# Layer norm's roots taken by way of DRAM, second-layer weight sums made early and kept in DRAM, operand forms moved to VectorE

## The reference

```
attn = softmax(masked q k^T / 8) v                     # 8 heads, local and strided masks
h = gelu(attn @ w_in);  u, v = halves of h
v_n = (v - mean) / sqrt(var + 1e-6) * g_ln
x = attn + (u * (w_sg @ v_n + b_sg)) @ w_out
mu, var = mean and variance of x over its 512 features
xn = (x - mu) / sqrt(var + 1e-6) * g_ln2               # the layer norm of the title
out = x + relu(xn @ w_ch1) @ w_ch2                     # 512 -> 2048 -> 512
```

## Time and profile before

| | |
|---|---|
| median of 3 runs | 750.08 us (749.67 to 751.82) |
| the profiled execution's own time | 746.97 us |
| its span, first to last instruction | 745.2 us |
| PE busy | 677.8 us (91%) |
| DVE, ACT, POOL busy | 551.9, 364.3, 272.4 us |
| mean granted TensorE clock | 0.966 |
| moved by DMA | 82.37 MB, 31.6% of 16 engines' span |

### The profile page before, as it was taken

How to read it: one execution, slowest core, us unless ns; L and a number is a source line. 1 busy time by engine, 2 the same in 40 slices (tenths; PEclk the granted TensorE clock), 3 DMA queues, 4 the chain that set the end, 5 groups by cost and what they waited for, 6 DMA issues and landing times.

```text
span 745.2 us, 14093 instructions
## 1 busy us (share of the span) xinstructions
PE 677.8 (91%) x5158; PEld 635.7 (85%) x5160; DVE 551.9 (74%) x1288; ACT 364.3 (49%) x896; POOL 272.4 (37%) x262
## 2 busy tenths in 40 slices
PE   8899999899989999994689599989966999999998
PEld 4579888898789889994579489989966999999997
DVE  6877967996799776864346557646679979799794
ACT  6756747485647643342253244334555444344441
POOL 1386332323142344755242233024993211212112
PEclk9999999999999999997799999999987999999999
DMA  8560016000700050051124221557540452724501
GB/s 299 196 216 1 1 56 226 1 1 2 279 1 2 2 178 1 29 184 60 49 72 132 92 80 64 188 195 256 177 136 31 159 191 65 286 67 179 190 29 48
DMA packets 41396, 82.37 MB, mean 111 GB/s; under 512 B 3440, under 2 KB 28912, under 8 KB 38640
## 3 DMA queue, kind: packets, MB, share of 16 engines
q1 hardware_dynamic: 41328, 81.48, 31.6%
HBM read 53.15 MB, written 28.31 MB: 109 GB/s over the span
## 4 chain that ended last, share of the span: by engine, by line
PE 57%; POOL 13%; issue 12%; DVE 10%; DMA 4%; ACT 3%; POOLq 0%; DVEq 0%; SPq 0%; ACTq 0%
PE pair L1693 9%; PE pair L1695 9%; PE pair L1694 9%; PE pair L1485 7%; PE pair L1487 7%; PE pair L1486 7%; DVE stage L1361 3%; PE pair L1509 3%; PE pair L1524 3%; PE pair L1542 2%; DMA hid_scratch<-stage 2%; POOL w_lo L481 2%; POOL acc L453 1%; DVE probs L1144 1%; DMA x_scratch<-res 1%
## 5 line engine op out<-in xcount | busy, mean ns | idle before, releaser
L1693 PE MATMUL pair<-xf_hi,w_hi 128*128 128x288 f32 x896 | 271.3, 303 | 26.9 <-POOL w_lo L481 6.8
L1694 PE MATMUL pair<-xf_lo,w_hi 128*128 128x288 f32 x896 | 268.5, 300 | 0.0
L1695 PE MATMUL pair<-xf_hi,w_lo 128*128 128x288 f32 x896 | 267.6, 299 | 0.0
L1693 PEld LDWEIGHTS pair<-xf_hi,w_hi 128*128 128x128 f32 x896 | 172.1, 192 | 31.1 <-issue 13.1
L1695 PEld LDWEIGHTS pair<-xf_hi,w_lo 128*128 128x128 f32 x896 | 172.8, 193 | 0.0
L1694 PEld LDWEIGHTS pair<-xf_lo,w_hi 128*128 128x128 f32 x896 | 172.4, 192 | 0.0
L1361 DVE TENSOR_TENSOR stage<-pair,stage 128x576 f32<-128x576 f32 x136 | 100.5, 751 | 65.0 <-PE pair L1695 32.7
L963 ACT ACTIVATE xf_hi<-res 128x576 fp32r<-128x576 f32 x140 | 94.1, 682 | 104.6 <-PE pair L1695 67.2
L522 DVE TENSOR_TENSOR xf_lo<-res,xf_hi 128x576 fp32r<-128x576 f32 x134 | 112.1, 854 | 26.3 <-ACT xf_hi L963 26.2
L1048 ACT ACTIVATE stage<-stage 128x576 f32<-128x576 f32 x64 | 43.5, 683 | 90.1 <-DVE stage L1361 90.0
L853 POOL TENSOR_TENSOR xr<-xr,stage 128x576 f32<-128x576 f32 x16 | 32.3, 2017 | 139.4 <-DVE stage L1361 139.4
(11 more groups left out here) (127 smaller groups left out, 1360.1 us busy)
## 6 DMA issues: line engine op xcount, KB each, us to landing
hid_scratch<-stage SPq DMA_DIRECT2D x64, 288.0 KB, 2.3
res<-hid_scratch SPq DMA_DIRECT2D x16, 1152.0 KB, 6.7
w_raw<-w_ff_dram SPq DMA_DIRECT2D x16, 512.0 KB, 3.8
v_sb<-vW_dram SPq DMA_DIRECT2D x16, 384.0 KB, 6.8
x_scratch<-res SPq DMA_DIRECT2D x4, 1152.0 KB, 5.1
xr<-x_scratch SPq DMA_DIRECT2D x16, 288.0 KB, 2.9
out_dram<-xr SPq DMA_DIRECT2D x16, 288.0 KB, 2.3
k_sb<-kT_dram SPq DMA_DIRECT2D x15, 304.0 KB, 6.7
```

The lines of the kernel that those rows point to most:

```text
L1693: pe.matmul(dst, wh, xh, start=(start and x == 0), stop=False)
L1694: pe.matmul(dst, wh, xl, start=False, stop=False)
L1695: last = pe.matmul(dst, wl, xh, start=False, stop=(stop and x == n - 1))
```

## The change

Four edits go together.

1. The variance leaves the chip's wide layout. ACT copies one row of the variance (1x288 for each half, `copy_variance`) instead of taking the root in all 128 partitions. POOL stores it to DRAM, loads it back as 96x6, adds epsilon and raises it to the power -0.5 in two small operations, stores the result and loads it spread over 128 partitions: four transfers for each norm, sixteen in all, issued by POOL. DVE's reciprocal is gone. The norms' last step is later: item 0's `normalise_x` is at the start of period 2, item 1's at the start of the last period, and those of items 2 and 3 both in lockstep 1 of the tile before they are used.
2. First-layer weights are loaded in parts: the blocks of P1 and P2 straight to their place (`f_raw`), that of P4 straight to its place, and the whole unit to `w_raw` for POOL's sums. All of it is issued ahead of the first hidden store.
3. The sums of second-layer weights are made by POOL in locksteps 4 to 11 in `w_raw` itself and stored to DRAM. In tile 3 each unit's P1 and P2 blocks are loaded as soon as P2 of the last lockstep that reads its place is done, and the rest, sums among it, after that lockstep.
4. All forms of x for the hidden layer and their splits are on DVE; POOL keeps four for the output layer.

Two statistics are one product later or earlier in PE's list. The diff, cut to its core:

```diff
-W_PLAIN = (P1, P2, P4)
-NPLAIN = len(W_PLAIN)
+W_FIRST = (P1, P2)
+NFIRST = len(W_FIRST)
+NREST = FORMS - NFIRST
+NSUMS = NREST - 1
...
-    place = {(1, P4): 0, (2, P1): 1, (2, P4): 2, (3, P7): 3}.get((q, i))
+    place = {(1, P4): 0, (2, P2): 1, (3, P1): 2, (3, P7): 3}.get((q, i))
...
-            if g >= UNITS:
-                engine.wait_ge(product_ready, ((B - 1) * LOCKSTEPS + u // 2 + 1) * FORMS)
-            elif u <= 1:
...
+            def load_raw(g):
                 if g >= 2:
-                    sp.wait_ge(plain_lo, g - 1)
-                    sp.wait_ge(w_sum, 4 * (g - 1))
+                    sp.wait_ge(w_sum, NSUMS * (g - 1))
                 sp.dma_start(w_raw[:, g % 2, :], w_ff[g]).then_inc(wff_in[g % 2], 16)
+
+            def load_first(g):
+                u = g % UNITS
+                if g < UNITS:
+                    wait_unit(sp, g)
+                else:
+                    sp.wait_ge(product_ready, ((B - 1) * LOCKSTEPS + u // 2) * FORMS + P2 + 1)
+                sp.dma_start(f_raw[u][:], w_ff[g, :, 0:NFIRST * BLOCK]).then_inc(f_in[u], 16)
+
+            def load_rest(g):
+                u = g % UNITS
+                if g >= UNITS:
+                    sp.wait_ge(product_ready, ((B - 1) * LOCKSTEPS + u // 2 + 1) * FORMS)
+                sp.dma_start(s_raw[u][:, 0:BLOCK], w_ff[g, :, NFIRST * BLOCK:(NFIRST + 1) * BLOCK]).then_inc(r_in[u], 16)
+                if g >= UNITS:
+                    sp.wait_ge(w2_stored, 16 * (u + 1))
+                    sp.dma_start(s_raw[u][:, BLOCK:NREST * BLOCK], sums_dram[u]).then_inc(r_in[u], 16)
+
+            def load_raw2(u):
+                if u == 0:
+                    sp.wait_ge(w_sum, NSUMS * UNITS)
+                else:
+                    sp.wait_ge(w2_sum, NSUMS * u)
+                sp.dma_start(w_raw[:, 0, :], w_ff[UNITS + u]).then_inc(w2_in, 16)
+
+            def store_sums(u):
+                sp.wait_ge(w2_sum, NSUMS * (u + 1))
+                sp.dma_start(sums_dram[u], w_raw[:, 1, :]).then_inc(w2_stored, 16)
...
-            for g in range(2, EARLY + 1):
-                load_unit(g)
+            for g in range(2, EARLY):
+                load_raw(g)
+                load_first(g)
+                load_rest(g)
+            for g in range(EARLY, EARLY + 2):
+                load_raw(g)
+                load_first(g)
+                load_rest(g)
             save_x(B - 1)
+            for g in range(EARLY + 2, UNITS):
+                load_raw(g)
+                load_first(g)
+                load_rest(g)
             for n in range(B):
                 for q in range(LOCKSTEPS):
                     m = n * LOCKSTEPS + q
-                    if n == 0 and q == 0:
-                        load_unit(EARLY + 1)
...
+                    if n == 0 and q == 3:
+                        load_raw2(0)
+                    if LOCKSTEPS < m <= LOCKSTEPS + UNITS:
+                        store_sums(m - LOCKSTEPS - 1)
+                        if m < LOCKSTEPS + UNITS:
+                            load_raw2(m - LOCKSTEPS)
+                    if n == B - 1 and q >= 1:
+                        load_rest(UNITS + 2 * q - 2)
+                        load_rest(UNITS + 2 * q - 1)
+                    if n == B - 1:
+                        load_first(UNITS + 2 * q)
+                        load_first(UNITS + 2 * q + 1)
...
+            def sum_second(u):
+                pool.wait_ge(w2_in, 16 * (u + 1))
+                if u == 0:
+                    pool.wait_ge(w_sum, NSUMS * UNITS)
+                else:
+                    pool.wait_ge(w2_stored, 16 * u)
+                add_blocks(pool, w_raw[:, 0, :], w_raw[:, 1, :], w2_sum, NSUMS * u)
+
+            def store_variance(n):
+                pool.wait_ge(var_copied, 2 * (n + 1))
+                pool.dma_start(var_dram[n:n + 1, :], norm_at(n)[0][0:1, :, :].rearrange("p h t -> p (h t)")).then_inc(var_stored, 16)
+
+            def load_variance(n):
+                pool.wait_ge(var_stored, 16 * (n + 1))
+                wait_past(pool, var_step, n)
+                pool.dma_start(var_c[:], var_dram[n].rearrange("(p x) -> p x", p=RP)).then_inc(var_in, 16)
+
+            def invert_roots(n):
+                pool.wait_ge(var_in, 16 * (n + 1))
+                wait_past(pool, pow_done, n)
+                pool.tensor_scalar(var_eps_c[:], var_c[:], EPS, None, ALU.add).then_inc(var_step, 1)
+                pool.wait_ge(var_step, n + 1)
+                wait_past(pool, rstd_stored, 16 * n)
+                pool.tensor_tensor(rstd_c[:], var_eps_c[:], half_c[:], ALU.pow).then_inc(pow_done, 1)
+                pool.wait_ge(pow_done, n + 1)
+                pool.dma_start(rstd_dram[n].rearrange("(p x) -> p x", p=RP), rstd_c[:]).then_inc(rstd_stored, 16)
+
+            def spread_rstd(n):
+                pool.wait_ge(rstd_stored, 16 * (n + 1))
+                if n == 1:
+                    pool.wait_ge(group_ready, (B - 1) * len(GROUPS))
+                to = gt[:, 0, :] if n == 1 else norm_at(n)[0][:].rearrange("p h t -> p (h t)")
+                pool.dma_start(to, rstd_dram[n:n + 1, :].broadcast_to([P, S])).then_inc(rstd_in, 16)
...
             def last_period(b):
-                pool.wait_ge(pv_ready, B * TWINS)
-                form_t3(pool, 0)
+                spread_rstd(1)
+                for g in range(2):
+                    sum_weights(g)
...
-                    if following < B and q == 3:
-                        form_t2(pool, following)
-                        split_form(pool, fill_of(following, P7))
-                        form_t1(pool, following)
-                        form_t4(pool, following)
-                        split_form(pool, fill_of(following, P3))
-                    if following == B and q >= 1:
-                        for g in (UNITS + 2 * q - 2, UNITS + 2 * q - 1):
-                            sum_weights(pool, g)
-                            split_plain(pool, g)
...
+                    if early and q == 0:
+                        sum_chunks(pool, r)
+                    if norm and q == 0:
+                        invert_roots(n + 1)
+                    if early and q == 1:
+                        split_sum(pool, r)
+                        sum_chunks(pool, r + 1)
+                    if early and q == 2:
+                        split_sum(pool, r + 1)
+                        sum_chunks(pool, r + 2)
+                        split_sum(pool, r + 2)
+                    if early and q == 3:
+                        sum_chunks(pool, r + 3)
+                        split_sum(pool, r + 3)
+                    if 0 <= u < UNITS:
+                        sum_second(u)
+                    if norm and q == 0:
+                        spread_rstd(n + 1)
+                    if early and q == 3:
+                        store_variance(n + 2)
...
+            def copy_variance(n, h):
+                r = 4 * n + 2 + h
+                act.wait_ge(stat_ready, r + 1)
+                if n == 1:
+                    act.wait_ge(xn_done, 2)
+                elif n == B - 1:
+                    act.wait_ge(xn_done, 2 * n)
+                act.activation(norm_at(n)[0][0:1, h, :], statistic_at(r)[0:1, :], ACT.Copy).then_inc(var_copied, 1)
...
-            def invert_root(n, h):
-                rstd = norm_at(n)[0]
-                dve.wait_ge(sd_done, 2 * n + h + 1)
-                dve.reciprocal(rstd[:, h, :], rstd[:, h, :]).then_inc(rs_done, 1)
-
             def normalise_x(n, h):
-                rstd = norm_at(n)[0]
-                dve.wait_ge(rs_done, 2 * n + h + 1)
+                dve.wait_ge(rstd_in, 16 * (n + 1))
+                dve.wait_ge(sq_done, (2 * n + h + 1) * KC)
+                wait_past(dve, xn_done, 2 * n + h)
...
+                if q == 3:
+                    split_form(dve, fill + 3)
+                if border:
+                    form_t1(dve, following)
                 c12(m)
+                if border:
+                    form_t4(dve, following)
+                    split_form(dve, fill + 4)
+                if last and q == 3:
+                    split_rest(dve, UNITS + 3)
+                c21(m)
...
+                if s in (0, 2, 4, 6):
+                    split_rest(dve, UNITS + 4 + s // 2)
```

438 lines of the change are left out of this document (223 added, 215 removed).

## The result

| | before | after |
|---|---|---|
| time, median of four runs each, us | 749.88 (749.55 to 751.82) | 729.78 (725.27 to 733.39) |
| ratio, 95% interval | | 0.9724, 0.9666 to 0.9782 |
| profiled execution, own time / span | 746.97 / 745.2 | 728.94 / 727.1 |
| DMA moved, MB | 82.37 | 98.26 |

A forecast was written before the change was run, and what follows sets the result against it. PE was taken as the engine to be fed before 568 us, losing 62.2 us to waits and slow clock. Terms -12.6 - 11.3 + 7 - 12.6 - 2 = -31.5 from 746.97 gave 715.5, plus 3.1 offset: 718.5 us, range 702 to 737.

The forecast's parts named there:

- Tile 0: Locksteps 1 to 3: earlier loads of units 6 and 7 cut the loss from 26.8 to 14.2 us, saving 12.6.
- where the clock holds it is 16.6: Upper case for the first tile's saving, without the 4 us of slow pace added for two gaps near 3.9.
- Tile 1: Second tile: shorter statistic waits and full clock cut the loss from 15.8 to 4.5 us, saving 11.3 (bounds 5 and 14).
- Tiles 2 and 3: Borders and transfers: loss grows from 4.0 to 11 us, 7 worse (bounds 2 and 14), with lockstep 11's gap becoming 5.5.
- The hops: Root's four POOL-issued transfers per norm, 2.5 us each, 10 in all, hidden before normalise_x with 5 us to spare.
- POOL's transfers are late: Rival, chance 0.15: at 5 us a hop, normalise_x stands 5 us in locksteps 5 and 9; 728.5 us in all.
- Output layer: Start of the output layer: both waits for second-layer weights go, loss 15.6 becomes 3, saving 12.6 us (bounds 8 and 14).
- Attention: Attention periods: less DVE work before first scores, less about 2.7 us of new waits; 2 us saved (bounds -4 and +6).
- a gap of up to 2.6 us costs itself: PE clock rule: such gaps add no slow pace, while gaps from 3.9 us up cost 3 to 6 us more.
- The first tile's stall only changes its name: Rival, chance 0.14: P1's copy behind its store is late by itself, so less is saved in the first two tiles; 733.5 us.
- slower: the stage store: Rival, chance 0.07: stage-1 stores land late in locksteps 4 to 15, PE idles 33.6 us and the gain is gone.
- The clock holds: Rival, chance 0.14: no gap reaches 3.9 us, so 4 and 3 us of slow pace don't come; 709 us.

The follow-up runs named there:

- e7: Changed kernel with the loads of first-layer units 6 and 7 late again, behind hidden stores of lockstep 0: 736.77 us, ratio 0.9825 to the kernel before.
- e10: Changed kernel with the statistics of the late items back in their old places (behind P1 and P4, not P2 and P1): 735.75 us, ratio 0.9805.
- e1: Changed kernel with the second half of normalise_x in locksteps 5 and 9 moved behind the last drain: 728.77 us, ratio 0.9697.
- e2: Changed kernel with GpSimd's sums of second-layer units 1 and 5 cut to 16 of 256 columns of a block: 727.32 us, ratio 0.9699.
- e0: The changed kernel timed again without edit, beside the kernel before: 732.52 us (727.91 to 738.09, six runs), ratio 0.9768.
- e6: Changed kernel with the early sums' transfers (raw second-layer loads, stores of sums) cut to 16 of 1024 columns: 725.85 us, ratio 0.9683.
- e9: Changed kernel with the four forms and the splits of P7 and P3 back on GpSimd at the three tile borders: 742.87 us, ratio 0.9887.
- e11: Changed kernel with five combined fixes, then hidden and x loads spread further and ScalarE's roundings of remainders moved later: 719.88 us, ratio 0.9594.
- e5: Changed kernel with the remainders of second-layer units 12 to 15 split in two pieces, the second four steps later: 734.24 us, ratio 0.9787.
- e3: Changed kernel with the remainders of second-layer units 14 and 15 split by GpSimd instead of VectorE: 731.7 us, median of five.
- e4: Changed kernel with three attention moves: first variance statistic one u group later, two normalise_x pieces later: 724.86 us, ratio 0.9669.

## Why the prediction was right, and where it was not

The time lies in the range, 11 us above the forecast's value and 3 above its own case (711 to 727), and terms were off on both sides. Tile 0 gained 4.3 us more than forecast, and tile 1 6.7, tiles 2 and 3 2.6, the output layer 5.9 and the attention 2.5 less. Only tile 0 offsets the others; it was the width of the range, 702 to 737, and not the terms, that made the hit.

*What bounds the kernel*: right. What moved lies ahead of 568 us, in PE's waits and the clock behind them; the rest took 138.2 us in both.

*Tile 0, 12.6 forecast, 16.9 measured.* The mechanism holds step by step. Unit 7 was to land at 328 to 331 (340.4 before) and ScalarE's rounding to come behind sums that end at 337 (345.81 before), and so they did:

```profile
329.56 0.75 POOL L482 TENSOR_TENSOR s_raw<-w_raw 128x256 f32<-128x256 f32 x1 [0.17 <-DMA w_raw<-w_ff_dram]
```

```profile
336.46 0.45 ACT L1028 ACTIVATE acc_hi<-acc 128x288 fp32r<-128x288 f32 x1 [2.13 <-POOL acc L464]
```

VectorE stands until 337.5 as forecast. The idle time is 6.5 us (1.88, 0.45, 0.94, 3.25) and not 10.2. The clock fell twice, behind 1.88 and behind 3.25, for 3.4 us each, so the slow pace of about 3.5 us came as forecast (4), and that the gain equals the bound "where the clock holds it is 16.6" is a coincidence: the clock did not hold. VectorE's stand behind the weight split, 3.4 us in the sum, cost 1.9. Wrong was that nobody but the roots waited for ACT's table loads: PE waited 1.96 us in lockstep 3 for a root behind one, and this wait went unpriced. e7 and e10 show the loads and the second mean's place as causes, with some 6.5 and 1.3 to 2.5 us; what the adds' order and the missing reciprocals add to that was not tried.

*Tile 1, 11.3 forecast, 4.6 measured: the step that failed.* The waits for statistics did shrink (3.91 to 0.94 and 0.26); where `normalise_x` holds PE up less, in e1 and e2, the second mean waits 2.44 and 2.43, which is the forecast's 2.3 to 2.7. But I left 4.5 us of loss for the tile and it has 11.2 (57.3 less 46.1), 8.0 of them idle. Two causes were not in the sum. Both halves of `normalise_x` stand in one lockstep with seven drains, and take 3.77 and 2.58 us beside GpSimd, where I counted two of 1.8 and no price for PE: gaps of 1.69 and 2.60 (e1, e2). And at the border VectorE's split is shut out by GpSimd's adds, 1.53. I had seen the contention on GpSimd's side (0.72 becoming 1.73) and not asked what it does to VectorE. The other 3.2 us are pace: the clock fell for 3.4 us behind the gap of 2.60, where I had put tile 1 at full clock.

*Tiles 2 and 3, +7 forecast, +9.6 measured (+12.8 in e0).* Lockstep 11 was right: 5.31 us of idle for 5.5, and the clock fell; e6 shows that the new megabyte makes 3.0 of it. What I had not counted are locksteps 9 and 10, 3.7 us over before, 3.2 of it gaps: `normalise_x` again, and roots that came late. The two borders there, 1 us each in the sum, cost nothing (locksteps 8 and 12 take 11.2).

*The hops: sized well and hidden in one tile out of two.* The four hops in tile 0's chain took 10.1 us (2.3, 1.9, 1.9 and 3.9) for the forecast's 10, and ended 6.7 us before VectorE took them up. In tile 1's chain they took 14.3 (1.8, 1.9, 4.0 and 6.5). Besides, GpSimd does sum 4, whose load lands at 442.2, ahead of the last hop, and VectorE idles 4.01 us in lockstep 9. The rival "POOL's transfers are late" is thus not refuted but small: PE waits 1.90 us behind it in after. In e9 and e11, where something was put ahead of it, PE waits 7.37 and 5.38. The two late hops had other transfers beside them (DMA engines 57% and 98% busy, and 25% during tile 0's first three). VectorE was busy 94% of the time during those three, which landed in 1.9 to 2.3 us, and 89% and 12% during the late two, so nothing here points to a port held by VectorE. That the other transfers are the cause is argued from this and not tried.

*Output layer, 12.6 forecast, 6.7 measured.* Both old waits went. The next late one stands where I put it, step 11, and is 4.17 us where the sum has 3.0 (1.4 and 1.6 for VectorE's start). Item 0 loses 9.4 us against the 44.8 of a later item, and not 3: 5.4 are idle, and the other 4 are slow pace, for which the sum has nothing, since a wait of 3.0 lay below the 3.9 it had read as the limit. The clock is at 0.50 for 6.9 us behind the wait; in e0 it is for 3.4 behind the same 4.17, and item 0 takes 51.7. The mis-sized term of the wait is VectorE's work: the remainder now spans five blocks, 1.48 us and not 1.2,

```profile
550.27 1.48 DVE L500 TENSOR_TENSOR w_lo<-s_raw,w_hi 128x1280 fp32r<-128x1280 f32 x1
551.67 1.42 DVE L540 TENSOR_TENSOR xf_lo<-res,xf_hi 128x576 fp32r<-128x576 f32 x2
553.01 1.49 DVE L500 TENSOR_TENSOR w_lo<-s_raw,w_hi 128x1280 fp32r<-128x1280 f32 x1
```

and VectorE waits 1.85 us more for a form that ScalarE rounds behind two remainders. In all it finished the last remainder 24.0 us after T (the end of the last hidden lockstep, 534.8), and not some 20.4. e5 and e3 show that the total binds: neither putting off a part of the work nor sharing it helped.

*Attention, -2 forecast, +0.5 to +7.7 measured.* The reciprocals went; the waits for sums, priced at 2.7 us in each of two periods, come to 5.0 (1.78 in period 1, 1.07 and 2.19 in period 2), about as priced; not priced was `normalise_x(1)` ahead of v, which cost PE 2.6. What I missed outright is the clock: the rule "a gap of up to 2.6 us costs itself", taken from one row, is wrong in nine of the ten profiles with the changed kernel's attention and in the trace of before itself (2.28 us, then 0.50), and that is the kernel's new spread. In e4, with these gaps fewer, the spread is half.

*The other rivals.* "The first tile's stall only changes its name" and "slower: the stage store" did not come; hidden stores landed in a median of 2.4 us. "The clock holds" did not come either, and its condition was no help: in tiles 0 and 1 no gap reached 3.9 us, and the clock fell three times.

## What to carry to other kernels

Price an operation on VectorE by what GpSimd does beside it, and the other way round, since each shuts the other out. A gap of PE of about 2 us may cost a slow stretch behind it as well (with the changed kernel's attention it did in nine of ten profiles at 2.2 us and in three at 1.8), so a kernel that waits less in sum may run faster and still spread more. When a large transfer is moved, list every small transfer and store that others wait for and see what it now stands behind: e11 mended one lockstep and lost more in another.

## What the runs showed of the hardware

- VectorE on two SBUF operands is shut out while GpSimd runs such operations back to back: 0.76 us became 3.22 beside four adds, 1.42 became 6.84 beside two splits of 1280 columns. With an operand in PSUM VectorE passed at 0.82 us an operation, and at 0.80 with GpSimd idle.
- The same gap of PE (2.18 and 2.19 us) left the clock at 2.4 GHz in one execution and took it to 1.2 GHz in another, for 1.5 us of time lost. Over ten profiles it fell behind 1.78 us in three, behind 2.15 to 2.19 in nine and behind 2.36 to 3.09 in six. In e4 it fell 1.5 us after a gap of 1.73 us, and stayed at 0.50 for 6.8 us, with a second gap of 1.05 us inside.
- A transfer of 2.2 KB issued by GpSimd takes it 0.5 to 0.6 us to issue and lands 1.6 to 2.3 us after the issue began in eleven of the twelve in after, and 3.2 to 4.4 us in e11's second chain, beside loads of 512 or 1152 KB and hidden stores.
- The table load of ACT ahead of a root takes 1.28 us, and PE waited for it in before (1.96 us in lockstep 3).
